# Order of VectorE and ScalarE within the turns of a sine-gated MLP: second reduction step behind the first, splits and bank copies behind the square

## The reference

```
h = x @ w_in            # x: 1536 x 512, w_in: 512 x 2048
g = h * np.cos(h)
return (g @ w_out)      # w_out: 2048 x 512
```

## Time and profile before

| | |
|---|---|
| median of 3 runs | 830.08 us (829.36 to 831.15) |
| profiled execution | 832.66 us |
| its span, first to last instruction | 830.7 us |
| TensorE busy | 802.8 us (97%) |
| VectorE busy | 611.7 us (74%) |
| ScalarE busy | 333.2 us (40%) |
| GpSimd busy | 399.1 us (48%) |
| mean granted TensorE clock | 0.995 |

### The profile page before, as it was taken

The page is one execution under the profiler, slowest core; times in us unless marked ns, Lnnn a source line. Parts: engine busy times, 40 slices in busy tenths (PEclk is TensorE's granted clock), DMA queues, the critical chain, the costliest instruction groups (busy, mean ns, idle before and its releaser), DMA issues.

```text
span 830.7 us, 11709 instructions
## 1 busy us (share of the span) xinstructions
PE 802.8 (97%) x4362; PEld 668.7 (80%) x4362; DVE 611.7 (74%) x924; ACT 333.2 (40%) x630; POOL 399.1 (48%) x357
## 2 busy tenths in 40 slices
PE   8999999999999999999999999988999999999997
PEld 7888888888888888888888888867877677786775
DVE  6987766766766766766766765788797787877886
ACT  4643222222222222222222222365667566675652
POOL 4875343343343343343343342547686675866721
PEclk9999999999999999999999999998999999999999
DMA  9842101111101111101101101000101101000003
GB/s 327 312 152 64 39 26 39 39 63 39 39 26 39 39 63 39 39 26 40 39 25 39 39 26 39 13 27 26 51 26 26 39 13 52 25 27 26 0 13 140
DMA packets 19868, 44.85 MB, mean 54 GB/s; under 512 B 2344, under 2 KB 2392, under 8 KB 19812
## 3 DMA queue, kind: packets, MB, share of 16 engines
q1 hardware_dynamic: 19812, 44.10, 16.4%
HBM read 40.93 MB, written 3.17 MB: 53 GB/s over the span
## 4 chain that ended last, share of the span: by engine, by line
PE 72%; DVE 13%; ACT 8%; issue 4%; DMA 1%; POOL 1%; SPq 0%; ACTq 0%; DVEq 0%
PE ps L1344 31%; PE ps L1325 27%; PE ps L1409 6%; DVE temps L1192 5%; PE ps L1402 4%; DVE temps L1186 3%; ACT temps L861 2%; ACT temps L842 1%; ACT w_hi L672 1%; PE ps L1242 1%; DMA att<-att_in 1%; PE ps L1292 1%; DVE x_lo L1003 1%; DVE y L1127 1%; DVE h_f L1127 1%
## 5 line engine op out<-in xcount | busy, mean ns | idle before, releaser
L560 POOL TENSOR_TENSOR h_lo<-temps,h_hi 128x512 fp32r<-128x512 f32 (+1 forms) x128 | 135.1, 1057 | 295.6 <-ACT h_hi L731 295.5
L731 ACT ACTIVATE h_hi<-temps 128x512 fp32r<-128x512 f32 (+1 forms) x128 | 67.2, 525 | 337.0 <-DVE temps L1015 337.0
L998 DVE TENSOR_TENSOR y<-ps,y 128x512 f32<-128x512 f32 x180 | 123.8, 688 | 71.8 <-PE ps L1344 71.8
L1344 PE MATMUL ps<-h_hi,w_hi 128*128 128x512 f32 x384 | 150.6, 392 | 0.1
L1325 PE MATMUL ps<-x_hi,w_lo 128*128 128x512 f32 (+1 forms) x448 | 150.6, 336 | 0.0
L1325 PE MATMUL ps<-x_hi,w_hi 128*128 128x512 f32 (+1 forms) x448 | 150.5, 336 | 0.1
L1325 PE MATMUL ps<-x_lo,w_hi 128*128 128x512 f32 (+1 forms) x448 | 150.6, 336 | 0.0
L1344 PE MATMUL ps<-h_lo,w_hi 128*128 128x512 f32 x384 | 150.4, 392 | 0.0
L1344 PE MATMUL ps<-h_hi,w_lo 128*128 128x512 f32 x384 | 149.4, 389 | 0.0
L1325 PEld LDWEIGHTS ps<-x_hi,w_hi 128*128 128x128 f32 x448 | 84.7, 189 | 12.8 <-DVE temps L1029 0.3
L1325 PEld LDWEIGHTS ps<-x_lo,w_hi 128*128 128x128 f32 x448 | 84.7, 189 | 11.7
(11 more groups left out here) (111 smaller groups left out, 1370.7 us busy)
## 6 DMA issues: line engine op xcount, KB each, us to landing
w_raw<-w_in SPq DMA_DIRECT2D x96, 256.0 KB, 2.6
att<-att_in SPq DMA_DIRECT2D x24, 512.0 KB, 7.2
temps<-p_scr SPq DMA_DIRECT2D x4, 768.0 KB, 4.2
out<-y SPq DMA_DIRECT2D x12, 256.0 KB, 2.2
att<-dp_in SPq DMA_DIRECT2D x1, 24.0 KB
p_scr<-att SPq DMA_DIRECT2D x1, 24.0 KB
lam<-lam_in SPq DMA_DIRECT2D x1, 6.0 KB, 1.8
```

The lines of the kernel that those rows point to most:

```text
L560: pool.tensor_tensor(hs_lo[side][:, f, at], ring(s, i), f32(hs_hi[side][:, f, at]), ALU.subtract).then_inc(s_hlo, 1)
L731: act.activation(hs_hi[s % SIDES][:, f, at], ring(s, i), ACT.Copy).then_inc(s_hhi, 1)
L998: dve.tensor_tensor(at, from_bank, at, ALU.add).then_inc(s_y, 1)
L1344: mm = pe.matmul(ps[:, DOWN_BANK + g % DOWN_BANKS, :], ww[:, s // SIDES % 2, f, at], hh[side][:, f, tokens], start=(f == 0 and n == 0), st ...
```

## The change

It reorders VectorE's and ScalarE's instructions in the turns of the MLP; no instruction is added or removed, and TensorE, GpSimd and SyncE keep their orders.

- VectorE: both steps of a turn stand together. Behind them come the evictions of part 3, then a gate (its own turn's for v < 4, the one before for v > 4), then the other evictions. Token sums move into `gate`. In turns 0 and 1 the last groups of the stage before and the splits of the last x chunk are placed anew.
- ScalarE: nothing stands between a turn's cast and its sine any more. Splits of gates and token sums, and copies out 0 and 1, come behind the square; copy-in 14 moves to turn 1 and copy-in 16 to behind turn 2's square; copies stand ahead of the splits.

```diff
--- before.py
+++ after.py
@@ -827,10 +827,6 @@
 
             for v in range(GATES):
                 q, m, j = QUARTERS + v // 6, v // 6, v % 6
-                if j == 2 and m:
-                    carry_in(m - 1, 14)
-                if j == 3 and m:
-                    carry_in(m - 1, 16)
                 act.wait_ge(s_g, v + 1)
                 if v == 0:
 
@@ -840,21 +836,6 @@
                 if v >= T_RING:
                     act.wait_ge(s_r2, v - T_RING + 1)
                 act.activation(kf[:, v % T_RING, :], ps[:, v % UP_BANKS, :], ACT.Copy, scale=INV_2PI).then_inc(s_k, 1)
-                if j == 0 and m:
-                    gate_high(m - 1, 8, 5)
-                if j in (1, 2):
-                    gate_high(m, j - 1, j - 1)
-                if m == FULL and j >= 3:
-                    gate_high(m, j - 1, j - 1)
-                elif j == 3:
-                    sum_high(m, 2, 0)
-                elif j == 4:
-                    gate_high(m, 3, 3)
-                    sum_high(m, 4, 1)
-                    carry_out(m, 0)
-                    carry_out(m, 1)
-                elif j == 5:
-                    gate_high(m, 7, 4)
                 act.wait_ge(s_r2, v + 1)
                 if v >= T_RING:
                     act.wait_ge(s_gate, v - T_RING + 1)
@@ -864,19 +845,36 @@
                 if v < 2:
                     x2_high(2, 2 * v)
                     x2_high(2, 2 * v + 1)
+                if j == 1 and m:
+                    carry_in(m - 1, 14)
                 if j == 2 and m:
                     carry_out(m - 1, 14)
+                    carry_in(m - 1, 16)
                 if j == 3:
                     if m:
                         carry_out(m - 1, 16)
                     carry_in(m, 0)
                     carry_in(m, 1)
+                if j == 4:
+                    carry_out(m, 0)
+                    carry_out(m, 1)
+
+                if j == 0 and m:
+                    gate_high(m - 1, 8, 5)
+                if j in (1, 2) or m == FULL and j:
+                    gate_high(m, j - 1, j - 1)
+                elif j == 3:
+                    sum_high(m, 2, 0)
+                elif j == 4:
+                    gate_high(m, 3, 3)
+                    sum_high(m, 4, 1)
+                    sum_high(m, 5, 2)
+                elif j == 5:
+                    sum_high(m, 6, 3)
+                    gate_high(m, 7, 4)
                 if m < FULL:
                     if j == (3 if m else 1):
                         w2_sums_high(m)
-                    if j == 4:
-                        sum_high(m, 5, 2)
-                        sum_high(m, 6, 3)
                     if j in (1, 2):
                         w1_piece(q + 1, j - 1)
                     if j in (4, 5):
@@ -1144,7 +1142,10 @@
                 dve.tensor_tensor(at, one, other, ALU.add).then_inc(s_comb, 1)
 
             def gate(v):
-                t = v % T_RING
+                t, m, j = v % T_RING, v // 6, v % 6
+                if m < FULL and j == 4:
+
+                    token_sum(m, 3, 3, t2[3], gate_of(m, 1), t2[2])
                 dve.wait_ge(s_sq, v + 1)
                 if v >= T_RING:
 
@@ -1158,25 +1159,18 @@
                         dve.wait_ge(s_glo, split_done(was, k))
                 dve.scalar_tensor_tensor(out=gg[:, t, :], in0=cs[:, t, :], scalar=1.0, in1=ps[:, v % UP_BANKS, :],
                                          op0=ALU.subtract, op1=ALU.mult).then_inc(s_gate, 1)
+                if m < FULL and j == 2:
+                    dve.wait_ge(s_gate, 6 * m + 3)
+                    token_sum(m, 0, 0, t2[0], gate_of(m, 2), gate_of(m, 0))
+                if m < FULL and j == 3:
+                    dve.wait_ge(s_gate, 6 * m + 4)
+                    token_sum(m, 1, 0, t2[1], gate_of(m, 3), gate_of(m, 2))
+                    token_sum(m, 2, 1, t2[2], gate_of(m, 3), t2[0])
 
             for v in range(GATES):
                 m, j = v // 6, v % 6
                 t = v % T_RING
                 bank = ps[:, v % UP_BANKS, :]
-                if v == 1:
-                    down(STEPS - 1, 0)
-                    down(STEPS - 1, 1)
-                if v == 2:
-                    down(STEPS - 1, 3)
-                if v:
-                    gate(v - 1)
-                if m < FULL and j == 3:
-                    dve.wait_ge(s_gate, 6 * m + 3)
-                    token_sum(m, 0, 0, t2[0], gate_of(m, 2), gate_of(m, 0))
-                if m < FULL and j == 4:
-                    dve.wait_ge(s_gate, 6 * m + 4)
-                    token_sum(m, 1, 0, t2[1], gate_of(m, 3), gate_of(m, 2))
-                    token_sum(m, 2, 1, t2[2], gate_of(m, 3), t2[0])
                 dve.wait_ge(s_k, v + 1)
                 if v == 0:
 
@@ -1185,24 +1179,27 @@
                     dve.wait_ge(s_sin, v - T_RING + 1)
                 dve.scalar_tensor_tensor(out=rr[:, t, :], in0=kf[:, t, :], scalar=-C1, in1=bank, op0=ALU.mult,
                                          op1=ALU.add).then_inc(s_r1, 1)
-                if v + 1 < GATES:
-                    second(v, 3)
-                    second(v + 1, 0)
                 dve.wait_ge(s_r1, v + 1)
                 dve.scalar_tensor_tensor(out=rr[:, t, :], in0=kf[:, t, :], scalar=-C2, in1=rr[:, t, :],
                                          op0=ALU.mult, op1=ALU.add).then_inc(s_r2, 1)
-                if m < FULL and j == 4:
-                    token_sum(m, 3, 3, t2[3], gate_of(m, 1), t2[2])
-                if v == 1:
-                    down(STEPS - 1, 2)
-                if v + 1 < GATES:
-                    second(v + 1, 1)
-                    second(v + 1, 2)
+                if v < 2:
+                    down(STEPS - 1, 2 * v)
+                if v < GATES - 1:
+                    second(v, 3)
+
+                if v < 4:
+                    gate(v)
+                elif v > 4:
+                    gate(v - 1)
+                if v < 2:
+                    down(STEPS - 1, 2 * v + 1)
+                    x2_low(2, 2 * v)
+                    x2_low(2, 2 * v + 1)
+                if v == GATES - 1:
+                    second(v, 3)
                 else:
-                    second(v, 3)
-                if v in (1, 2):
-                    x2_low(2, 2 * v - 2)
-                    x2_low(2, 2 * v - 1)
+                    for part in range(3):
+                        second(v + 1, part)
                 if m == FULL and j == 1:
                     dve.wait_ge(s_y2, added_count(FULL - 1, 3))
                     dve.wait_ge(s_y3, carried_count(FULL - 1, 1))
```

## The result

| | before | after |
|---|---|---|
| median | 830.62 us (4 runs, 829.36 to 835.51) | 863.03 us (4 runs, 862.79 to 864.26) |
| ratio after/before | | 1.0382, 95% interval 1.0338 to 1.0425 |
| profiled execution | 832.66 us | 864.26 us |
| its span | 830.7 us | 862.4 us |
| mean granted TensorE clock | 0.995 | 0.986 |

What follows compares the result with a forecast made beforehand. ScalarE's own queue was taken to bound the MLP pass: 15.5 + 11.7 pieces + 8.7 second steps + 1.8 waits = 37.7 us against 34.5. Over all passes +21.7 us, so 852 us, range 838 to 861.

Steps and rivals of the forecast that it cites:

- behind: ScalarE's time per pass from the end of the square's share to the next cast; pieces priced 7.1 before, 11.7 after, plus waits.
- Part 1: VectorE's second step right behind the first: six evictions leave the chain between cast and sine, -3.1 us a pass.
- Part 2: Seven token splits and two copies out leave ScalarE's wait and stand ahead of the next cast: +4.6 us a pass.
- Part 3: The six second steps, lengthened by GpSimd's low splits, were to sum to 8.67 us a pass, as before: 0.
- R: Duration of VectorE's second step, or its sum over a pass's six turns; alone 0.69 us, longer under a GpSimd instruction.
- (a): New wait: eviction of group 5 behind turn 0's second step delays the up product and the cast of turn 1: +0.54.
- (b): New wait: copy into bank 14, behind turn 1's square, needs group 11 evicted: +1.16 us.
- (c): New wait: gate 4's split on ScalarE waits 0.08 for its gate, behind eviction and token sum.
- the edge that the forecast named: Turn 0's second step starts 0.24 before gate 4's split ends; later, R is 1.84, +1.05 a pass, time 859.
- Pass 0: First MLP pass: turn 4's first step behind gate and token sums, plus token splits and copies of turns 4, 5: +3.9.
- Last pass: Few splits, TensorE-bound in the middle; second steps ahead of evictions and sums bring the last gate earlier: -1.5 us.
- TensorE's clock falls: Rival: TensorE gaps of 7 us in pass 0 and nearly 3 later bring 1.2 GHz; unhidden 862 us; chance 0.06.

Runs made afterwards that it cites:

- e1: Kernel before with ScalarE's new order only, VectorE keeping its old one; 855.89 us, ratio 1.0311.
- e11: Kernel before with only the second step moved right behind the first, the six evictions behind both; 831.45 us, ratio 1.0021.
- e6: Changed kernel with the splits of gates and token sums back between cast and sine, one turn later than their gate; 839.22 us, ratio 1.0106.
- e3: Changed kernel with the second weight split of turn 5 ahead of gate 4's split instead of behind it; 854.94 us, ratio 1.0306.
- e9: Changed kernel with token splits, weight splits and copies out 14, 16, 0, 1 between cast and sine; copies in 14, 16 stay behind squares; 831.69 us, ratio 1.0037.

## Why the prediction was right or wrong

- **What bounds: right for the changed kernel, incomplete for the one before.** Where ScalarE's loop sets the pass, "behind" is the priced pieces and the waits: 7.1 before, 11.7 in e1 with no wait, 13.8 in the changed kernel with 11.7 and some 2 of waits. But in the kernel before another loop, over the banks and TensorE, is about as long: e11 takes 3.1 us out of ScalarE's and the pass keeps its 34.4. Two readings of the earlier trace rows were short too: 2.0 of TensorE's 3.2 us (34.5 - 31.3) are waits for a bank in that view (1.4 for evictions, 0.6 for a copy-in), not nearly all, and ScalarE has one more wait in the pass, 0.3 us for gate 0 between cast and sine, where it costs nothing.
- **Part 1, evictions -3.1: right as a term** (e1 has 3.1 between the steps, after has none). It is not a gain for itself (e11).
- **Part 2, moved pieces +4.6: right.** e1: 7.1 to 11.7. e6 takes most of it back.
- **Part 3, R of 8.67 unchanged: wrong by 1.0**, in turn 0 alone; five of six second steps were within 0.03. The rule (ends 0.55 behind the GpSimd instruction) held in every row that shows that instruction singly; its input was 0.24 us off.
- **Part 4: (a) 0.54 was 0.5 to 0.6; (b) 1.16 was 1.1 idle, 1.2 from start to start; (c) is the step that failed.** "Gate 4's split waits 0.08" was 0.3 (736.78 less 735.96 + 0.52). I took the gate at the 0.60 that neighbours on VectorE stand apart, and did not price its semaphore wait for the token sum just ahead (0.81 apart). The 0.2 us are themselves lost, and they push turn 0's second step across the edge that the forecast named, 0.24 away: +1.05. Together 1.25 us in each of passes 1 to 6 and about 1.0 in the last one, 8.5 of the 10 us by which the sum of the spans was short. e3 takes both out of ScalarE's way and lands on 37.7, 36.3 and 854.9.
- **Pass 0, +3.9: right** (4.0), the two token sums ahead of turn 4's first step included (1.66 and 1.74 us under GpSimd's splits). Its gap of TensorE was forecast at 7 us and is 6.87; no run takes its other terms apart:

```profile
575.01 0.80 PE L1406 MATMUL ps<-x_hi,w_hi 128*128 128x512 f32 x1 [6.87 <-ACT h_f L826]
```

- **Last pass, -1.5: wrong, +0.8.** One us is turn 0's second step (e3's last pass is 45.7 us, after's 46.7). Of the rest, one piece is to be seen: the two combined sums ahead of turn 5's first step run into a GpSimd split and take 3.43 us, against 2.45 for the pair before them (838.86 to 841.34). The other 0.3 us have no reading. I had walked this pass coarsely.

```profile
844.37 3.43 DVE L1142 TENSOR_TENSOR y<-y,h_f 128x1024 f32<-128x1024 f32 x2
...
844.60 2.13 POOL L610 TENSOR_TENSOR x_lo<-temps,x_hi 128x512 fp32r<-128x512 f32 x1 [5.85 <-ACT x_hi L797]
```

- **The rival "TensorE's clock falls": its mechanism came, its price did not.** The gap before group 3 is 2.74 us in every pass from 2 on. In pass 2 the clock stays, in pass 3 it falls (0.50, the lower level of 1.2 GHz, from 693.0 to 694.5), and the passes are 38.98 and 38.93 us long. TensorE's timeline at the two stalls of either pass, and two stretches behind the gaps (15 matmuls in 3.0 us at 1.00, 9 in 2.5 us at 0.65):

```profile
651.48 0.50 PE L1406 MATMUL ps<-x_hi,w_hi 128*128 128x512 f32 x1 [2.74 <-ACT h_f L826]
658.93 0.50 PE L1399 MATMUL ps<-x_hi,w_hi 128*128 128x512 f32 x1 [2.38 <-DVE temps L1160]
...
690.46 0.50 PE L1406 MATMUL ps<-x_hi,w_hi 128*128 128x512 f32 x1 [2.74 <-ACT h_f L826]
697.87 0.50 PE L1399 MATMUL ps<-x_hi,w_hi 128*128 128x512 f32 x1 [0.72 <-DVE temps L1160]
```

```profile
653.00:656.00 3.00, 3.00 (x15) 2.47 (x14) 1.45 (x2) 1.48 (x3) 3.00 (x3) 1.00 0.00 0
...
693.00:695.50 2.50, 2.50 (x9) 1.98 (x8) 1.98 (x2) 0.45 (x1) 2.25 (x2) 0.65 0.00 0
```

  The lower clock costs TensorE 2.38 - 0.72 = 1.7 us, and it is taken out of the next wait, for gate 4. The time that the forecast gave this rival, 862, is near the measured one by chance: e3 has as low a clock (0.984 against 0.986) and 854.9.
- **The range** ended at 861 because this edge was priced alone, at 859; with the 0.2 us behind it and the last pass the same case gives 852 + 10 = 862.

## What to carry to other kernels

When instructions leave a wait that the engine has anyway, count each as added work; when a chain is shortened by pushing evictions back, follow the bank they free to the next product before booking the gain. Where the duration of an instruction jumps on who starts first, price its neighbours' semaphore waits within an engine too, and if the margin is smaller than what is left unpriced, forecast both sides. A ledger of one loop only holds while the other loops have slack: on a balanced kernel, check the second-longest loop for each gain.

## What the runs showed of the hardware

- An instruction of VectorE that waits on a semaphore of the one right ahead of it starts later than one that doesn't, and not by one amount. Neighbours without such a wait start 0.60 apart (each 0.68 or 0.69 long). A first and a second step start 0.72 apart (0.71 to 0.73 in all 48 turns of the changed kernel), a gate and a token sum that reads it the same (14 times); token sum 3 and gate 4 start 0.81 apart, all seven times (735.25 to 736.06; 691.41 to 692.22 in e3). Why this pair takes 0.09 more is open, and no run took its semaphore wait away.
- A second step that starts together with GpSimd's split of a weight, within 0.02, takes 1.84 us, in passes 1 to 7 of the changed kernel alike; 0.31 ahead of that split, in e3, it takes 0.89. Nearer than some 0.02 the recorded starts don't tell the outcome: e11 has 0.69 and 1.84 at the same recorded distance (above).
- The granted clock falls after gaps of TensorE much shorter than the 5.66 us of the earlier trace rows, and not each time. In the changed kernel the gap of 2.74 us brings it in pass 3 and not in pass 2 (above). In e6 a gap of 1.83 us stands in each of passes 2 to 6, and the granted clock of the 3 us behind it is 1.00, 0.73, 0.52, 1.00 and 0.65; after e11's gap of 1.74 us it stays at 1.00. The Trainium skill (TensorE: Matmul & The Clock Gate, Part 1: The HAM clock gate) has a TensorE that was idle fall back to 1.2 GHz; what these traces add is that one and the same gap did so in one pass and not in another. The stretches behind the gaps of passes 3 and 5 of e6:

```profile
679.92:683.00 3.08, 3.08 (x10) 2.46 (x11) 3.05 (x5) 3.00 (x6) 1.39 (x2) 0.73 0.00 0
...
750.77:754.00 3.23, 3.23 (x14) 2.67 (x15) 3.20 (x5) 3.00 (x6) 1.54 (x2) 1.00 0.00 0
```

- What such a fall costs depends on what else is short. The five passes of e6 are 35.50, 35.85, 35.41, 35.04 and 35.83 us long, which is not the order of their clocks and prices nothing. The four executions of the changed kernel have a mean clock of 0.984 to 0.988 and lie within 1.5 us, in no order of the clock either. In e9, where TensorE is nearly without slack, the twelve executions go with it: 830.2 to 831.9 us for the eight at 0.994 or 0.996, 833.5 at 0.992, 835.1 at 0.990, 837.5 and 837.9 at 0.988. No run changed the clock alone.
